# Wider PSUM tiles for y in a fused recurrent attention and two-layer FFN kernel, and a new order of its first two periods

## The reference: what is computed

```python
f = 1.0 / (1.0 + np.exp(-f_logit))
for t in range(S):
    state = f[:, :, t, :, None] * state + np.einsum('bhd,bhe->bhde', k[:, :, t], v[:, :, t])
    y[:, :, t] = np.einsum('bhd,bhde->bhe', q[:, :, t], state)
```

## Time and profile before

| | |
|---|---|
| median of three runs | 997.84 us (995.43 to 998.28) |
| profiled execution | 997.89 us, its span 995.9 us |
| TensorE matmul busy | 961.6 us (97%), 11972 records |
| VectorE, ScalarE, GpSimd busy | 495.5, 391.1, 277.4 us |
| mean granted TensorE clock | 0.995 |

### The profile page before, as it was taken

How to read it: one execution, slowest core, us unless ns; L and a number is a source line. 1 busy time by engine, 2 the same in 40 slices (tenths; PEclk the granted TensorE clock), 3 DMA queues, 4 the chain that set the end, 5 groups by cost and what they waited for, 6 DMA issues and landing times.

```text
span 995.9 us, 27529 instructions
## 1 busy us (share of the span) xinstructions
PE 961.6 (97%) x11972; PEld 820.2 (82%) x11972; DVE 495.5 (50%) x700; ACT 391.1 (39%) x685; POOL 277.4 (28%) x221
## 2 busy tenths in 40 slices
PE   5789989999999999999999999999999999999998
PEld 4668767887888778788878879999999999999997
DVE  5878675575657666573325663333333333333332
ACT  2735633443534343453444453232332332322322
POOL 2236454454536454444423541000000000000000
PEclk9989999999999999999999999999999999999999
DMA  6743313303030212111003321000010000000000
GB/s 204 211 124 93 107 40 109 86 14 96 35 98 22 77 55 77 60 50 50 2 2 109 97 76 68 1 33 32 1 63 0 32 32 0 32 32 0 32 1 32
DMA packets 54187, 56.88 MB, mean 57 GB/s; under 512 B 19520, under 2 KB 46400, under 8 KB 54080
## 3 DMA queue, kind: packets, MB, share of 16 engines
q1 hardware_dynamic: 51232, 43.86, 15.4%
q10 hardware_dynamic: 2848, 11.44, 3.1%
HBM read 45.84 MB, written 9.44 MB: 56 GB/s over the span
## 4 chain that ended last, share of the span: by engine, by line
PE 90%; DVE 3%; issue 3%; ACT 2%; DMA 2%; ACTq 0%; DVEq 0%
PE ps L1536 8%; PE ps L1535 8%; PE ps L1540 8%; PE ps L1574 7%; PE ps L1573 7%; PE ps L1577 7%; PE ps L1183 6%; PE ps L1071 6%; PE ps L1206 5%; PE ps L1185 5%; PE ps L1192 5%; PE ps L1208 5%; PE ps L1212 5%; PE ps L1133 2%; PE ps L1106 1%
## 5 line engine op out<-in xcount | busy, mean ns | idle before, releaser
L1489 DVE TENSOR_TENSOR g<-g 128x512 f32<-128x512 f32 x96 | 67.1, 699 | 264.0 <-ACT g L1409 264.0
L1409 ACT ACTIVATE g<-ps 128x512 f32<-128x512 f32 x112 | 67.1, 599 | 284.6 <-PE ps L1540 280.3
L669 POOL TENSOR_TENSOR glo<-g,ghi 128x512 fp32r<-128x512 f32 x80 | 111.2, 1390 | 234.7 <-ACT ghi L502 234.7
L876 DVE SCALAR_TENSOR_TENSOR g<-e,g 128x512 f32<-128x512 f32 x80 | 63.0, 788 | 142.6 <-ACT g L496 142.6
L1535 PE MATMUL ps<-xhi,wts 128*128 128x512 f32 x336 | 131.9, 393 | 0.7 <-ACT xhi L487 0.7
L1536 PE MATMUL ps<-xhi,wts 128*128 128x512 f32 x336 | 131.9, 393 | 0.0
L1574 PE MATMUL ps<-wts,ghi 128*128 128x384 f32 x380 | 128.9, 339 | 0.0
L1573 PE MATMUL ps<-wts,ghi 128*128 128x384 f32 x380 | 127.6, 336 | 0.0
L495 ACT ACTIVATE e<-ps 128x512 f32<-128x512 f32 x80 | 47.8, 598 | 166.1 <-PE ps L1192 166.1
L1183 PE MATMUL ps<-xhi,wts 128*128 128x512 f32 x240 | 99.6, 415 | 0.7 <-ACT g L496 0.7
L1540 PE MATMUL ps<-xlo,wts 128*128 128x512 f32 x336 | 95.3, 392 | 0.0
(11 more groups left out here) (123 smaller groups left out, 1576.4 us busy)
## 6 DMA issues: line engine op xcount, KB each, us to landing
raw<-w SPq DMA_DIRECT2D x52, 192.0 KB, 2.6
q<-qk SPq DMA_DIRECT2D x22, 256.0 KB, 4.4
gate<-fl SPq DMA_DIRECT2D x10, 512.0 KB, 5.0
k<-qk SPq DMA_DIRECT2D x10, 512.0 KB, 3.7
x<-xo ACTq DMA_DIRECT2D x6, 768.0 KB, 3.3
xs<-x ACTq DMA_DIRECT2D x6, 768.0 KB, 4.3
out<-PT SPq DMA_DIRECT2D x24, 192.0 KB, 1.9
v<-vn SPq DMA_DIRECT2D x11, 384.0 KB, 3.6
```

What stands on the lines that cost most here:

```text
L669: nc.gpsimd.tensor_tensor(out=glo[:, f % 2, :], in0=g[:, f % 2, :], in1=ghi[:, f % 2, :].bitcast(F32), op=ALU.subtract).then_inc(s_glo, 1)
```

## The change

The three functions that write y get tiles of 64 partitions where a head begins at an even block (four heads of eight), and keep two of 32 where it begins at an odd one. `q_state` has 12 products for 16, a half of `values` 24 for 32, `last_column` 16 for 24. The wide ones come first, then the narrow ones. TensorE's two hand-written periods deal the feeds out anew; the end of the levels of (1,0) moves from the second period into the end of the first, and the third group of (1,1) gets two feeds behind it for one. VectorE and ScalarE swap neighbouring steps in the same periods.

```diff
-    def shares(group):
-        for m in range(KD):
-            a, third = divmod(4 * m + group, 3)
-            for j in range(2):
-                if third == 1 or third == 2 * j:
-                    yield m, a, j, third
+    def shares(j):
+        def tiles(a):
+            first, n = 3 * a + j, 32 if (3 * a + j) % 2 else 64
+            return [(a, *divmod(32 * i, P), n, 32 * i - 96 * a) for i in range(first, first + 2, n // 32)]
+        return [tiles(j) + tiles(j + 2), tiles(1 - j) + tiles(3 - j)]
...
# ScalarE, first_period
+            krow_copy(1, 0)
             high(1, 7)
-            krow_copy(1, 0)
# ScalarE, second_period
             ffn_step(8)
+            y_copy(1, 0)
             hidden_copies(1, 9)
-            y_copy(1, 0)
...
             ffn_step(12)
+            take6(1, 1)
             hidden_copies(1, 13)
-            take6(1, 1)
...
# VectorE, first_period
             ffn_step(0)
-            q_update(1, 0, 1)
-            rest(1, 0, 1)
+            step(1, 0, 1)
             activate(1, 1)
-            q_update(1, 0, 2)
-            activate(1, 2)
-            rest(1, 0, 2)
-            split_weights(split_at(1, 2))
-            q_update(1, 0, 3)
+            step(1, 0, 2)
+            ffn_step(2)
+            step(1, 0, 3)
             activate(1, 3)
-            rest(1, 0, 3)
             q_update(1, 0, 4)
-            activate(1, 4)
             q_update(1, 1, 0)
             rest(1, 0, 4)
+            activate(1, 4)
             rest(1, 1, 0)
# VectorE, second_period
             state_update(1, 0)
-            ffn_step(9)
+            activate(1, 9)
             q_update(1, 1, 4)
-            activate(1, 10)
             q_update(1, 2, 0)
             rest(1, 1, 4)
+            activate(1, 10)
             rest(1, 2, 0)
...
-            ffn_step(12)
+            activate(1, 12)
             q_update(1, 1, 6)
-            activate(1, 13)
             q_update(1, 2, 2)
             rest(1, 1, 6)
             rest(1, 2, 2)
-            q_update(1, 2, 3)
+            activate(1, 13)
+            step(1, 2, 3)
             activate(1, 14)
-            rest(1, 2, 3)
# TensorE, q_state
             for i in range(2):
-                for group in range(4):
-                    for j in range(2):
-                        m, a, _, third = [x for x in shares(group) if x[2] == j][i]
+                for both in zip(shares(0)[i], shares(1)[i]):
+                    for j, (a, m, at, n, channel) in enumerate(both):
                         u, rows = j ^ part, slice(HP * j, HP * j + D)
                         last = nc.tensor.matmul(
-                            pair(c, h, "Y")[32 * group:32 * group + 32, u, m * CELL:m * CELL + C],
-                            state[rows, 2 * (h % 2) + u, 2 * a * D + 32 * third:2 * a * D + 32 * third + 32],
+                            pair(c, h, "Y")[at:at + n, u, m * CELL:m * CELL + C],
+                            state[rows, 2 * (h % 2) + u, 2 * a * D + channel:2 * a * D + channel + n],
...
# TensorE, values
-            for i in range(4):
-                for group in range(4):
-                    m, a, j, third = list(shares(group))[i]
+            for i, j in ((0, 0), (0, 1), (1, 0), (1, 1)):
+                for a, m, at, n, channel in shares(j)[i]:
...
-                            banks[32 * group:32 * group + 32, u, m * CELL + HP * z:m * CELL + C],
-                            vz[rows, h % 2, z, a, 32 * (third + j):32 * (third + j) + 32], blocks,
+                            banks[at:at + n, u, m * CELL + HP * z:m * CELL + C],
+                            vz[rows, h % 2, z, a, channel + 32 * j:channel + 32 * j + n], blocks,
...
# TensorE, last_column
-                for block in range(4 * KD):
+                for block, n in ((0, 64), (6, 64), (4, 64), (10, 64), (2, 32), (3, 32), (8, 32), (9, 32)):
...
# TensorE, first_period
             feed(1, 0, (1,))
             product(1, 0, 1)
-            feed(1, 0, (3,))
-            feed(1, 0, (4, 5))
+            feed(1, 0, (3, 4))
             product(1, 0, 2)
-            feed(1, 0, (6, 7))
+            feed(1, 0, (5, 6))
             product(1, 0, 3)
-            feed(1, 0, (8, 9))
+            feed(1, 0, (7, 8))
             group(1, 0, 0)
-            feed(1, 0, (10, 11, 12))
+            feed(1, 0, (9, 10, 11))
             group(1, 0, 1)
-            feed(1, 0, (13, 14))
+            feed(1, 0, (12, 13))
             group(1, 0, 2)
-            feed(1, 0, (15,))
+            feed(1, 0, (14, 15))
+            end_of_levels(1, 0)
# TensorE, second_period
-            feed(1, 1, (0,))
-            end_of_levels(1, 0)
-            feed(1, 1, (1, 2))
+            feed(1, 1, (0, 1))
             y_and_state(1, 0)
-            feed(1, 1, (3,))
+            feed(1, 1, (2,))
             end_of_y(1, 0)
-            feed(1, 1, (4, 5))
+            feed(1, 1, (3, 4))
             group(1, 1, 0)
-            feed(1, 1, (6, 7, 8))
+            feed(1, 1, (5, 6, 7))
             group(1, 1, 1)
-            feed(1, 1, (9, 10, 11))
+            feed(1, 1, (8, 9, 10))
             group(1, 1, 2)
-            feed(1, 1, (12,))
+            feed(1, 1, (11, 12))
             end_of_levels(1, 1)
```

More of the change, by code:

```diff
@@ L1099, in q_state @@
                 pe.wait_ge(s_u, count(c, h, 1, 1))
-            begun_groups = set()
             for i in range(2):
-                for group in range(4):
-                    for j in range(2):
-                        m, a, _, third = [x for x in shares(group) if x[2] == j][i]
+                for both in zip(shares(0)[i], shares(1)[i]):
+                    for j, (a, m, at, n, channel) in enumerate(both):
                         u, rows = j ^ part, slice(HP * j, HP * j + D)
                         last = nc.tensor.matmul(
-                            pair(c, h, "Y")[32 * group:32 * group + 32, u, m * CELL:m * CELL + C],
-                            state[rows, 2 * (h % 2) + u, 2 * a * D + 32 * third:2 * a * D + 32 * third + 32],
+                            pair(c, h, "Y")[at:at + n, u, m * CELL:m * CELL + C],
+                            state[rows, 2 * (h % 2) + u, 2 * a * D + channel:2 * a * D + channel + n],
                             queries(c, h)[rows, u * PAIRS + a, 0:C],
-                            start=(part == 0 and (u, group) not in begun_groups), stop=False, skip_group_check=True)
-                        begun_groups.add((u, group))
+                            start=(part == 0 and i == 0), stop=False, skip_group_check=True)
             if part:
@@ L1133, in values @@
                         last = nc.tensor.matmul(
-                            banks[32 * group:32 * group + 32, u, m * CELL + HP * z:m * CELL + C],
-                            vz[rows, h % 2, z, a, 32 * (third + j):32 * (third + j) + 32], blocks,
-                            start=(fresh and z == 0 and i == 0), stop=(z == 1 and i == 3), skip_group_check=True)
+                            banks[at:at + n, u, m * CELL + HP * z:m * CELL + C],
+                            vz[rows, h % 2, z, a, channel + 32 * j:channel + 32 * j + n], blocks,
+                            start=(fresh and z == 0 and (i, j) == (0, 0)), stop=(z == 1 and (i, j) == (1, 1)),
+                            skip_group_check=True)
             if z:
@@ L1162, in last_column @@
             for u in range(UB):
-                for block in range(4 * KD):
-                    m, group = divmod(block, 4)
+                for block, n in ((0, 64), (6, 64), (4, 64), (10, 64), (2, 32), (3, 32), (8, 32), (9, 32)):
+                    m, at = divmod(32 * block, P)
                     a = block // 3
-                    last = nc.tensor.matmul(pair(c, h, "Y")[32 * group:32 * group + 32, u, m * CELL + C:(m + 1) * CELL],
-                                            state[:, 2 * (h % 2) + u, 32 * block:32 * block + 32],
+                    last = nc.tensor.matmul(pair(c, h, "Y")[at:at + n, u, m * CELL + C:(m + 1) * CELL],
+                                            state[:, 2 * (h % 2) + u, 32 * block:32 * block + n],
                                             q_last[:, h % 2, u * PAIRS + a:u * PAIRS + a + 1],
```

## The result

The changed kernel took 1008.73 us (median of four executions, 1007.92 to 1011.25), the kernel before 996.63 us on the same chip (995.22 to 998.28): a ratio of 1.0125, 95% interval 1.0097 to 1.0153. It is slower by 12 us. 1004.3 was forecast, with a range of 996 to 1011. The profiled execution took 1008.0 us, with a span of 1006.2.

What follows compares the result with a forecast made beforehand. TensorE, busy 97% of the span, was taken to bound the kernel. 997.9 us profiled + 9.1 (tiles, ten units) + 0.3 (first two units) - 3.0 (order) = 1004.3 us, range 996 to 1011.

Steps and rivals of the forecast that it cites:

- The other reading of the forecast: Level-5 block before a level-1 block: 64 records took 0.69 us, 0.50 scaled by columns, so a shape change costs 0.19.
- +0.13: `last_column`, per unit: 16 wide products at 29 ns and 16 narrow at 10 make 0.62 us for 0.49.
- -0.18: Second half of `values`, per unit: 16 wide and 32 narrow records take less than the 0.70 us of before.
- the term of +0.3: First two units, without `q_state`: borders +1.4 us together, shortened instruction gaps may offset them; +0.3 (-1.5 to +1.5).
- Rival 1: Wide tiles in y: record sets the time, borders free, up to 7.9 us saved in ten units; 987 to 991; chance 0.13.
- Rival 2: Borders cost half (0.07 us), 0.5 per unit, and the order brings its 3.0: 1000.2 us; chance 0.17.
- Net -2.6, and half of the 0.71 gap: Two reordered periods: 7.1 us go, 4.5 come, plus half the instruction gap at 154.0: -3.0 us (-8 to +2).
- (a): First period, level 2: reached at 65.7, level-1 query update ends at 66.8; new wait 1.0 us, 0.3 more at level 3.
- (b): First period, third group: gate sigmoid delays H5's high part and the key updates behind it; new wait 2.1 us.
- (c): `last_column`: TensorE arrives 6.8 us after H8, not 8.4, while the state update ends 8.2 after; new wait 1.1 us.
- the clock's 1.5 us: Second period: granted clock at 0.50 after two waits slows eight transposes and four FFN matmuls; 1.5 us counted as gone.
- Rival 3: Borders as forecast, order brings nothing: wait (b) halves the clock, further wait of 1 to 2 us; 1008; chance 0.2.

Runs made afterwards that it cites:

- few_borders: Kernel before with the wide tiles, old orders, and products of one width issued together (5 borders in a unit for 8): 999.23 us, ratio 1.0040.
- the two extra products: Kernel before plus one unread one-column product in the middle of each half of `q_state`: 997.12 us with 32 columns of weights, 1004.15 with 64.

## Why the prediction was right, and where it was not

**The tiles: right, by a mechanism that the runs confirm, and with luck in the sum.** 9.4 us were forecast (9.1 and 0.3) and 9.0 measured. Its signs came: TensorE busy from 200 to 300 us, each block of y in two rows with a pause of 0.17 to 0.20 between, `last_column` at 1.0. Within the sum some sizes were off and made up for each other.
- A border was put at 0.12 us, nearest to one pair of rows; by itself, in `q_state`, it costs 0.17 to 0.18, and over the unit 0.15. The other reading of the forecast, from level 5 against level 4, has an error: 0.71 us scaled to two thirds of the columns is 0.47, not 0.50, so that reading gives 0.22 and not 0.19, too much. The rule of the Trainium skill, "TensorEngine Tiling (Array Packing)", Key Properties, that a change of the tiling mode drains the engine, is borne out: two kernels that differ by nothing but a product's width differ by 7.0 us.
- The tiles' own work was put at -0.05 us (+0.13 and -0.18) and comes out at nothing. The +0.13 of `last_column` was right: 0.12, with wide loads 27 ns apart where 29 were taken, and the 0.62 us forecast for its work, with one border of 0.17, are the 0.80 of few_borders. The -0.18 was mis-sized: the second half of `values` got 0.08 longer with a border of 0.17 in it, so its own work is -0.09.
- So a unit costs 1.18 us, not 0.91, and ten would be 11.8. The first two units were mis-sized the other way: from the first new state to the first feed the kernel before takes 12.1 us (44.54 to 56.63), the changed one 10.0 (45.27 to 55.26) and the wide tiles alone 9.4 (45.80 to 55.21), so the term of +0.3 was -2.1 to -2.7 in the profiled executions. And in the steady units the profile shows less than 1.18: over the six periods from 189 us on, 279.3 us for 274.5, +4.8 where 6 x 1.18 = 7.1. The rest is in the kernel before, whose periods were 45.4 but for 46.27 and 46.66; in these stand pauses that no operand explains, in the middle of a product's loop and of `values` (its timeline of TensorE):

```profile
350.01 0.65 PE L1071 MATMUL ps<-q,k 48*62 48x32 f32 x30 [0.61 <-issue]
...
420.43 0.38 PE L1133 MATMUL ps<-PT,vz 64*32 64x128 f32 x2 [0.93 <-issue]
```

The changed kernel's periods are all 46.52 to 46.57 there. Its instructions are fewer (81 transfers of instructions for 86), and such pauses fell out of its middle. The forecast allowed for this only in the first two units, within its 1.5 us either way, and in the 0.71 us at 154. That the shorter code is the reason is argued, not shown: the kernels that differ little in code have the pauses at other places too.

**Rival 1, that records set the time and borders are free, is out** by the two extra products and by the steady period. The Trainium skill's rule of some 60 cycles for a matmul ("TensorEngine Tiling (Array Packing)", Instruction Overhead), by which `last_column` would have saved a third, doesn't hold here: its 48 narrow records take 0.49 us, 10.2 ns or 24 cycles of 2.4 GHz each (49 for a product of two records), and with a third fewer of them it takes 0.80 us with one border and 1.01 with three. **Rival 2**, borders at half price and 0.5 us a unit, is out too, with 1.18.

**The order: the sign was wrong.** The failing step is "Net -2.6, and half of the 0.71 gap: -3.0". The step took three waits for the whole price and the half clock for gone, and put TensorE's arrival at the third group 1 us too late. What was said to go went, 5.6 us of waits and the half clock at 142; alone, in the second period, this brings 3.3 us. What was said to come came as well, at the three places and for the reasons named. (a) was 0.95 for 1.0, and the 0.3 at level 3 didn't come. (b) was 2.05 and then 1.00, 3.05 in all for 2.1: the key updates were ready at 92.9 and 94.55, nearly as forecast (93.2 and 94.5), but TensorE stood at the third group at 90.9 (92.96 - 2.05) and not at 91.9. (c) was 1.39 for 1.1. One more of 0.49 wasn't foreseen. In all 5.9 for 4.5. And the clock's 1.5 us, credited as gone, was not gone but moved: the windows above lose 15 x 0.23 + 20 x 0.09 = 5.3 us of full clock in the changed kernel from 90 to 125 us, for 40 x 0.04 = 1.6 before. Waits -5.6 + 5.9 and clock -1.6 + 5.3 are +4.0. What the order costs in runs is 3.1 us beside the wide tiles (1008.73 against 1005.64, not clear of noise), and 5.4 and 4.4 beside the narrow ones (clear of it both times). The text's own sign of failure showed too: entry into chunk 2, wrong if later than 157 us, came at 161.4. By itself it proves little, since the executions profiled differ: it came at 160.90 and 158.94 in the two profiles of the order with narrow tiles, and at 161.95 with wide tiles and the old order.

**The clock goes with the spread, not with the sign.** Rival 3 had this mechanism, and its 1008 is the number nearest to the result: no gain by the order, and the clock falling after wait (b). But the clock behind that wait falls in some executions only. The same code, both orders with narrow tiles, was profiled twice, with 1.86 and 1.00 us of wait at the third group the first time and 1.47 and 1.00 the second; its windows from 90 us, first and second time:

```profile
90.00:105.00 15.00, 12.14 (x198) 9.76 (x197) 9.31 (x14) 5.55 (x10) 9.00 (x6) 0.89 0.13 41
```

```profile
90.00:105.00 15.00, 12.53 (x206) 10.21 (x206) 10.52 (x16) 6.06 (x12) 9.41 (x7) 1.00 0.19 64
```

Its ten executions took 999.1 and 999.5 us at a mean clock of 0.996 and 0.997, 1001.5 to 1003.4 at 0.991 to 0.993 (five), and 1000.7 to 1003.3 at 0.974 to 0.976 (three); the kernel before took 994.8 to 997.4 at 0.996 and 0.997. At equal clock the order costs some 3 to 4 us, by two executions only, and where the clock is lower, 2 to 4 more.

**What stays open.** The two halves of the order don't add (+4.0 and -3.3 alone, +4.4 to +5.4 together), though in the profiled executions they nearly do: the new state of unit (1,1) begins 4.8 us later with the first half, 1.8 earlier with the second and 3.1 later with both, but only 1.3 later in the repeat. Which part of the rest is clock could not be told, since a profile shows one execution. So the best order of the first period isn't known either: the gates behind `take5` brought 4.2 us, but made a wait elsewhere.

**The sum.** The forecast was 4.4 us low. The order is 6.1 of that (-3.0 forecast, +3.1 measured beside the wide tiles); the tiles take back 0.4 (9.4 and 9.0) and the starting time 1.3 (997.9 profiled, 996.6 the median). The total was near because its largest term, the tiles, came out right, and that was in part luck: units dearer than forecast (1.18 us for 0.91) and pauses of the kernel before that vanished made up for each other.

## What to carry to other kernels

Count the changes of tile shape before counting products: a border inside a stream of small tiles cost 0.10 to 0.18 us, as much as 10 to 17 of the records around it, so one shape throughout, or all tiles of one shape together, comes before fewer and wider tiles. Where an order is moved by one feed, waits that go are easier to see in a profile of before than those that come, so the latter deserve the wider bound; and each half of such a reordering should be tried alone: here that found 3.3 us which the whole had hidden.

## What the runs showed of the hardware

- A border between 32- and 64-column tiles costs 0.17 to 0.18 us in the middle of `q_state`, where one product of 64 columns among narrow ones pays it twice, and 0.10 in `last_column`, where the borders stand eight records apart (0.21 us for two). In `q_state` and `values` it shows as 0.17 to 0.20 us in which no weights are loaded. One more product of the same width costs 0.02 us per unit for four records.
- In `last_column` 16 records with loads of 128 rows by 64 columns follow 27 ns apart and take some 0.12 us more than the 32 narrow ones that they replace (10.2 ns each); `new_state`'s loads of 128 rows by 48 columns take 25 ns each.
- After two waits of 1 to 2 us among small products the granted clock fell to 0.50 (1.2 GHz) for some microseconds in one execution and not in another of the same code: a mean of 0.89 and of 1.00 from 90 to 105 us.
- A low clock in the first 44 us, of which TensorE is busy for 28, cost nothing that could be seen: the kernel with wide `values` and the second period's new order was profiled with a mean clock of 0.979 in its fastest execution, 991.2 us, while its executions at 0.994 to 0.998 took 992.7 to 997.3, six of seven of them up to 994.0 (another at 0.978 took 995.4). In the kernel before, ten executions at 0.979 had a median of 994.8 us and forty at 0.995 to 0.997 one of 995.7; where their clock was low is not known. The window of the profiled one:

```profile
0.00:44.00 44.00, 28.39 (x908) 24.82 (x912) 32.42 (x52) 22.24 (x36) 13.69 (x19) 0.61 0.76 231
```
